# Channel attention and a Strassen-Winograd FFN: products chained in two PSUM banks, output blocks handled singly, token sums made by adding DMAs

## The reference

```python
qn = q / (np.linalg.norm(q, axis=1, keepdims=True) + 1e-06)
kn = k / (np.linalg.norm(k, axis=1, keepdims=True) + 1e-06)
s = kn.transpose(0, 2, 1) @ qn / tau
a = softmax(s)                       # over the last axis, 1e-9 added to the sum
x = (v @ a).reshape(12032, 256)
h = x @ w_in                         # w_in (256, 2048)
g = h * (1.0 / (1.0 + np.exp(-h)))
out = g @ w_out                      # w_out (2048, 256)
```

## Time and profile before

| | |
|---|---|
| median of 3 runs | 1074.42 us (1074.38 to 1074.58) |
| span of the profiled execution | 1072.1 us |
| PE busy | 1067.7 us, 4848 matmuls |
| VectorE busy | 730.0 us |
| ScalarE busy | 633.9 us |
| GpSimd busy | 62.0 us |
| DMA | 54.08 MB, mean 50 GB/s |

### The profile page before, as it was taken

One profiled execution on the slowest core, in us unless ns is written; L12 is line 12 of the kernel. 1 busy time (PEld: TensorE's weight loads), 2 busy tenths in 40 slices (PEclk: granted clock), 3 DMA queues, 4 the chain that ended last, 5 costly groups with the idle time before them and its releaser, 6 DMA issues.

```text
span 1072.1 us, 13055 instructions
## 1 busy us (share of the span) xinstructions
PE 1067.7 (100%) x4848; PEld 902.5 (84%) x4848; DVE 730.0 (68%) x941; ACT 633.9 (59%) x789; POOL 62.0 (6%) x33
## 2 busy tenths in 40 slices
PE   9999999999999999999999999999999999999998
PEld 8988888888888888888999888888888888888998
DVE  6889787567566566566788776667567566566665
ACT  7998665555555555555666655555555555555554
POOL 3792000000000000000000000000000000000000
PEclk9999999999999999999999999999999999999999
DMA  9991000200200200200200200200200200200100
GB/s 358 397 362 40 1 1 1 79 1 1 79 1 0 78 0 0 73 0 0 79 1 1 74 1 1 79 1 1 79 1 1 78 0 0 73 0 0 40 1 35
DMA packets 26365, 54.08 MB, mean 50 GB/s; under 512 B 2512, under 2 KB 6864, under 8 KB 26320
## 3 DMA queue, kind: packets, MB, share of 16 engines
q1 hardware_dynamic: 25888, 52.86, 13.5%
q10 hardware_dynamic: 432, 0.62, 0.2%
HBM read 41.16 MB, written 12.32 MB: 50 GB/s over the span
## 4 chain that ended last, share of the span: by engine, by line
PE 99%; DMA 0%; SPq 0%; ACT 0%; issue 0%
PE ps_o L530 16%; PE ps_o L531 16%; PE ps_o L529 16%; PE ps_h L496 14%; PE ps_h L495 14%; PE ps_h L494 14%; PE ps_o L434 5%; PE ps_o L449 1%; PE ps_o L456 1%; DMA qk<-k_dram 0%; PE ps_h L486 0%; PE ps_h L488 0%; PE ps_h L487 0%; PE ps_o L487 0%; PE ps_o L486 0%; PE ps_o L488 0%
## 5 line engine op out<-in xcount | busy, mean ns | idle before, releaser
L496 PE MATMUL ps_h<-b_hi,a_lo_rest 128*128 128x512 f32 (+1 forms) x504 | 194.1, 385 | 0.0
L495 PE MATMUL ps_h<-b_lo,a_hi_rest 128*128 128x512 f32 (+1 forms) x504 | 194.1, 385 | 0.0
L494 PE MATMUL ps_h<-b_hi,a_hi_rest 128*128 128x512 f32 (+1 forms) x504 | 194.0, 385 | 0.0
L978 DVE TENSOR_TENSOR h_b<-ps_h,u 128x512 f32<-128x512 f32 x96 | 66.4, 692 | 162.2 <-PE ps_h L496 162.1
L956 DVE TENSOR_TENSOR u<-ps_h,u 128x512 f32<-128x512 f32 x96 | 66.4, 692 | 142.4 <-PE ps_h L496 91.2
L750 ACT ACTIVATE h_a<-ps_h 128x512 f32<-128x512 f32 x96 | 57.4, 598 | 162.6 <-PE ps_h L496 162.6
L530 PE MATMUL ps_o<-g_lo_a,wo_hi 128*128 128x512 f32 (+1 forms) x384 | 147.9, 385 | 0.0
L529 PE MATMUL ps_o<-g_hi_b,wo_hi 128*128 128x512 f32 (+1 forms) x384 | 147.9, 385 | 0.0
L531 PE MATMUL ps_o<-g_hi_b,wo_lo 128*128 128x512 f32 (+1 forms) x384 | 147.9, 385 | 0.0
L529 PE MATMUL ps_o<-g_hi_a,wo_hi 128*128 128x512 f32 (+1 forms) x384 | 147.9, 385 | 0.0
L530 PE MATMUL ps_o<-g_lo_b,wo_hi 128*128 128x512 f32 (+1 forms) x384 | 147.8, 385 | 0.0
(11 more groups left out here) (138 smaller groups left out, 1602.1 us busy)
## 6 DMA issues: line engine op xcount, KB each, us to landing
v_raw<-v_t_dram SPq DMA_DIRECT2D x40, 256.0 KB, 3.7
out_t_dram<-v_raw SPq DMA_DIRECT2D x20, 512.0 KB, 3.2
qk<-q_dram SPq DMA_DIRECT2D x17, 384.0 KB, 10.8
qk<-k_dram SPq DMA_DIRECT2D x17, 384.0 KB, 11.8
wp_raw<-q_dram SPq DMA_DIRECT2D x7, 384.0 KB, 10.4
wp_raw<-k_dram SPq DMA_DIRECT2D x7, 384.0 KB, 11.8
w_in_raw<-w_in_dram SPq DMA_DIRECT2D x4, 512.0 KB, 11.8
wo_raw<-w_out_dram SPq DMA_DIRECT2D x4, 512.0 KB, 12.3
```

The lines of the kernel that those rows point to most:

```text
L494: nc.tensor.matmul(ps_h[:, bank, 0:n], w_hi, x_hi, start=start, stop=False, skip_group_check=True)
L495: nc.tensor.matmul(ps_h[:, bank, 0:n], w_hi, x_lo, start=False, stop=False, skip_group_check=True)
L496: return nc.tensor.matmul(ps_h[:, bank, 0:n], w_lo, x_hi, start=False, stop=stop, skip_group_check=True)
```

## The change

**Products.** p1 goes into bank X. ScalarE copies bank X into bank Y, still in PSUM ("seed"). p6 is then added upon p1 in bank X and gives U; p2 is added in bank Y and gives C11. ScalarE copies U out of bank X, p5 is added upon it and gives W, which is copied too, and p3 upon that gives the negative of C12. p7 starts bank Y anew; VectorE adds W and gets the negative of C22. p4 is added there, and VectorE adds U: C21. The signs of the weight sums are turned for it, and Silu takes a scale of -1 where the block is negative. Two of VectorE's five adds of a PSUM bank are left.

**Output blocks.** Each of C11, C12, C21 and C22 has its own tile, its own Silu, rounding, split and semaphores (`hi`, `lo`, `used`), and each output block of 3 matmuls stands alone between the products. The output banks are copied out one at a time at pairs 0 and 1.

**Token sums.** All token sums are now pure additions. For step 0 GpSimd makes them as before; for the others SP loads seven tiles of `x_raw` instead of four, and GpSimd issues seven DMAs that add a block of `v_t` from DRAM to a tile, in three rounds with a wait between.

**Code.** The loops over the steps are written out. In the last step of a batch ScalarE and VectorE take 448 columns in place of 512.

```diff
-BANK_P1, BANK_P6, BANK_P5, BANK_P7 = range(4)
+BANK_X, BANK_Y = range(2)
...
             def load_v(step):
+                places = ((T3, 0, 1), (B11, 0, 0), (B21, 1, 0), (B22, 1, 1))
+                if step:
+                    places += ((T1, 0, 0), (T2, 0, 0), (T4, 0, 0))
...
+            def add_tokens(step):
...
+                pool.wait_ge(v_loaded, 112 * step + 64)
+                add(T4, 0, 1).then_inc(t_first, 16)
+                add(T2, 0, 1).then_inc(t_first, 16)
+                add(T1, 0, 1).then_inc(t_first, 16)
+                add(T3, 1, 1).then_inc(t_first, 16)
+                pool.wait_ge(t_first, 64 * step)
+                add(T4, 1, 1).then_inc(t_second, 16)
+                add(T2, 1, 1).then_inc(t_second, 16)
+                pool.wait_ge(t_second, 32 * step)
+                add(T4, 1, 0).then_inc(t_third, 16)
...
+                p1(n, pair, par, tok)
+                output(n - 1, 0, 0, H12)
+                output(n - 1, 1, 0, H22)
+                p6(n, pair, par, tok)
+                p2(n, pair, par, tok)
+                output(n - 1, 0, 1, H12)
+                p5(n, pair, par, tok)
+                output(n - 1, 1, 1, H22)
+                p7(n, pair, par, tok)
+                output(n - 1, 0, 0, H11)
+                p3(n, pair, par, tok)
+                output(n - 1, 1, 0, H21)
+                p4(n, pair, par, tok)
+                output(n - 1, 0, 1, H11)
+                output(n - 1, 1, 1, H21)
+
+            def opening_pair():
+                pe.wait_ge(v_split, 3)
+                pe.wait_ge(a_split, 1)
+                p1(0, 0, 0, TOK)
+                pe.wait_ge(probs_split, 2)
+                fold(1, 0)
+                fold(1, 1)
+                p6(0, 0, 0, TOK)
+                p2(0, 0, 0, TOK)
+                fold(1, 2)
+                p5(0, 0, 0, TOK)
+                fold(1, 3)
...
+            def seed_u1(n, tok):
+
+                act.wait_ge(p1_done, n + 1)
+                if n:
+                    act.wait_ge(c21_made, n)
...
+                nc.scalar.activation(ps_h[:, BANK_Y, 0:tok], ps_h[:, BANK_X, 0:tok], ACT.Copy).then_inc(u1_seeded, 1)
...
+            def pair_step(n):
...
+                if n > 1:
+                    silu_c21(n - 1, before)
+                round_h(n - 1, before, H21, silu_21)
+                seed_u1(n, tok)
+                if it and pair == 0:
+                    copy_out(it - 1, 1, 0)
+                if it and pair == 1:
+                    copy_out(it - 1, 0, 1)
+                if it == 0 and pair < PAIRS - 1:
+                    round_a(0, pair + 1)
+                if it < ALL - 1 and pair == 3:
+                    round_t12(it + 1, 1 - par)
+                if it < ALL - 1 and pair == 4:
+                    round_v(it + 1, 1 - par)
+                if it < ALL - 1 and pair == 6:
+                    round_t34(it + 1, 1 - par)
+                copy_u(n, tok)
+                silu_c11(n, tok)
+                copy_w(n, tok)
+                if it and pair == 0:
+                    copy_out(it - 1, 1, 1)
+                silu_c22(n, tok)
+                silu_c12(n, tok)
+                round_h(n, tok, H22, silu_22)
+                round_h(n, tok, H12, silu_12)
+                if it and pair == 0:
+                    copy_out(it - 1, 0, 0)
+                round_h(n, tok, H11, silu_11)
+                place = n - PAIRS * (STEPS - 1)
+                if place in reload_at:
+                    old = reload_at[place]
+                    act.wait_ge(p4_done, PAIRS * (STEPS - 1) + old + 1)
+                    round_a(1, old)
...
+                make_c22(n, tok)
+                split_h(n, tok, H22)
+                if n == 0:
+                    split_wo(PARTS - 1)
+                make_c21(n, tok)
+                split_h(n, tok, H12)
+                if it == 0 and pair < PAIRS - 2:
+                    sum_a(0, pair + 2)
```

More of the change, by code:

```diff
@@ L36 @@
 FACTORS = 7
-BANK_P1, BANK_P6, BANK_P5, BANK_P7 = range(4)
+BANK_X, BANK_Y = range(2)
+H11, H12, H21, H22 = range(4)
 def channel_attention_ffn(nc, q, k, v_t, tau, w_in, w_out, out_t):
@@ L323, in _ @@
                 n = tokens_of(step)[1]
-                for late, t in enumerate((1, 0)):
-                    sp.wait_ge(out_copied, 2 * step + late + 3)
+                for t in (1, 0):
+                    for c in range(CK):
+                        sp.wait_ge(out_copied[CK * t + c], step + 1)
                     sp.dma_start(out_half(step, t), out_sb[:, t, :, 0:n]).then_inc(out_stored, 16)
@@ L424, in _ @@
             split_t34()
+            for step in range(1, ALL):
+                add_tokens(step)
         @block.tensor
@@ L580, in _ @@
-            for free in (o1_done, o2_done):
-                pe.sem_inc(free, 1)
+                x_hi, x_lo = b_hi[par][:, t, 0:tok], b_lo[par][:, t, 0:tok]
+                out = ps_h[:, bank, 0:tok]
+                nc.tensor.matmul(out, w_hi, x_hi, start=start, stop=False, skip_group_check=True)
+                nc.tensor.matmul(out, w_hi, x_lo, start=False, stop=False, skip_group_check=True)
+                return nc.tensor.matmul(out, w_lo, x_hi, start=False, stop=True, skip_group_check=True)
@@ new lines, in p4, with output @@
+            def p4(n, pair, par, tok):
+                pe.wait_ge(c22_made, n + 1)
+                product(pair, par, tok, BANK_Y, A22, T4, False).then_inc(p4_done, 1)
+            def output(n, f, c, g, stop=False):
+                it, pair = divmod(n, PAIRS)
+                tok = tokens_of(it)[1]
+                t = g % 2
+                if f == 0 and pair == 0:
+                    if it:
+                        pe.wait_ge(out_copied[CK * t + c], it)
+                    else:
+                        pe.wait_ge(wp_copied, 2 * FOLDS)
+                        pe.wait_ge(wo_split, PARTS)
+                pe.wait_ge(lo[g], n + 1)
+                block_, d = 2 * pair + f, slice(c * P, (c + 1) * P)
+                out = ps_o[:, CK * t + c, 0:tok]
+                last = pair == PAIRS - 1 and f == 1
+                nc.tensor.matmul(out, wo_hi[:, block_, d], g_hi[:, g, 0:tok], start=(pair == 0 and f == 0), stop=False,
+                                 skip_group_check=True)
+                nc.tensor.matmul(out, wo_hi[:, block_, d], g_lo[:, g, 0:tok], start=False, stop=False,
+                                 skip_group_check=True)
+                mm = nc.tensor.matmul(out, wo_lo[:, block_, d], g_hi[:, g, 0:tok], start=False, stop=last,
+                                      skip_group_check=True)
+                if c == 1:
+                    mm.then_inc(used[g], 1)
+                if c == 0 and last:
+                    mm.then_inc(out_summed[t], 1)
@@ L583, in _, with closing_outputs @@
+            def closing_outputs(n):
+                output(n, 0, 0, H12)
+                output(n, 1, 0, H22)
+                output(n, 0, 1, H12)
+                output(n, 1, 1, H22)
+                output(n, 0, 0, H11)
+                output(n, 0, 1, H11)
+                output(n, 1, 0, H21)
+                output(n, 1, 1, H21)
             pe.wait_ge(consts_made, 1)
@@ new lines, in silu_c12, with silu_c22, silu_c21 @@
+            def silu_c12(n, tok):
+                act.wait_ge(p3_done, n + 1)
+                if n:
+                    act.wait_ge(lo[H12], n)
+                nc.scalar.activation(h[:, H12, 0:tok], ps_h[:, BANK_X, 0:tok], ACT.Silu, scale=-1.0).then_inc(
+                    silu_12, 1)
+            def silu_c22(n, tok):
+                act.wait_ge(c22_made, n + 1)
+                nc.scalar.activation(h[:, H22, 0:tok], h[:, H22, 0:tok], ACT.Silu, scale=-1.0).then_inc(silu_22, 1)
+            def silu_c21(n, tok):
+                act.wait_ge(c21_made, n + 1)
+                nc.scalar.activation(h[:, H21, 0:tok], h[:, H21, 0:tok], ACT.Silu).then_inc(silu_21, 1)
```

533 lines of the change are left out of this document (221 added, 312 removed).

## The result

The changed kernel takes 1177.11 us (median of 4 runs, 1173.12 to 1183.39), the kernel before 1074.40 in the same series: a ratio of 1.096, interval 1.093 to 1.100. Forecast were 1085.3 and a range of 1079 to 1118. The direction was right, the size was too small by a factor of nine, and the range did not hold it.

The account below looks back on a forecast made before the run. The prediction held the feed-forward part bound by TensorE's matmul pace, so the change could only open gaps. Terms 6.9 + 1.1 + 1.7 + 1.2 + 0 = 10.9 us on 1074.4 gave 1085.3 us, range 1079 to 1118.

Parts of the forecast that it names:

- the sums made by DMAs: Token sums of eleven steps by adding DMAs: two rounds take 9.1 us at plain-load pace, 10.5 available, cost nought.
- the far bound, 77 us: Adds at twice the plain-load time, 18.2 us, cost 7.7 us in each of ten steps.
- the deadline of 33.0: Latest time into a step, in us, for ScalarE to begin rounding T1 and T2.
- the rival: Adds land late: 13.6 us, 3 late in each of ten steps, blocking ScalarE and p5; 30 us, 1115 us; chance 0.30.
- Reload: Second batch's weight roundings on ScalarE delay the seed copy and p6 at eight pairs, 0.85 us each: 6.9 us.
- The wide pair: Steady wide pairs: room 0.08 us before p6 and 0.01 before H12's first output; cost nothing.
- a rival at 0.12: Wide pairs stall too: 0.1 us missing in each of 79 pairs, 8 us more, 1093 us; chance 0.12.
- the narrow pairs: From p3's reader to the split of H12, 0.05 to 0.07 us late, 16 times: 1.1 us.
- Step 0's roundings: A weight rounding ahead of token roundings delays the copy of u for p5: 0.25, 0.25 and 0.67, sum 1.2 us.
- The opening: First pair: fold waits 1.0 us for the probabilities, late last folding copy 0.7; sum 1.7, between 1.0 and 3.
- Not slower: Rival: all waits met if ScalarE passes between instructions some 0.9 us a pair sooner; 1074 to 1076 us; chance 0.05.
- faster: Rival: fewer PSUM reads shorten the matmul pace by 3 ns each, 13 us, giving 1072 us; chance 0.03.

Follow-up runs that it names:

- hold10: Changed kernel without the adding DMAs, with ten extra 512-column ScalarE copies before the rounding of T1 and T2 in ten steps: 1175.19 us, ratio 1.094.
- Before_adds: Kernel before, loops written out, with the change's seven loads and seven adding DMAs a step in place of VectorE's token sums: 1088.55 us, ratio 1.014.
- mended: Changed kernel, T1/T2 rounded two pairs later, eight weight roundings behind the next seed copy, C22's first output block before C12's: 1087.65 us, ratio 1.012.
- seed_first: mended with ScalarE's seed copy moved ahead of the rounding of H21: 1085.18 us, ratio 1.010.

## Why the prediction failed, step by step

**The failed step: the sums made by DMAs, costed at nought.** The prediction bounded two rounds of adds between 9.1 and 18.2 us, allowed them 10.5, and took "the near end, nought, since the nearest row is the plain load of the same bytes". Measured are 15.8. Two things went wrong in this one step, the time of the rounds and the price of being late, and a third was right.

First the choice of the end. The nearest row moved the same bytes with another operation, and only the lowest 1.4 us of a range of 9.1 fitted the budget of 10.5. Even plain copies from GpSimd take 6.31 + 3.92 = 10.2, which the row's 9.1 had already missed by 1.1. With no row for an operation, and a penalty on one side only, nought was the edge of the range, not its middle. The prediction had worked out the far bound, 77 us, and given late adds 0.30, but left that part out of its range. The budget was slightly too large as well: the loads had landed 23.7 us into step 1 (213.00 less the step's start near 189.3, which is the p1 of its fourth pair at 219.90 less the 30.6 of three) where 22.5 was forecast, while ScalarE stood ready at 228.58 - 6.79 = 221.79, or 32.5, half a microsecond before the deadline of 33.0. From 23.7 to 33.0 are 9.3 us, and 15.8 is 6.5 late; the gap in PE there is 6.1, ScalarE's wait 6.8. So the arithmetic of the rival was right: with 15.8 in place of its 13.6 it gives 53 us by the budget of 10.5 and 65 by that of 9.3, and the ten gaps sum to 60.3. Its own middle, 1115 us, was still 62 below the measured time.

The Trainium skill's rule from "Collectives: The Full Stack", "The bandwidth ceiling: the fold count and why AG ≠ RS ≠ AR", that an add reads twice for each write and runs near half rate (there it is the reducing step of a ring of cores), was set against the row and lost. The runs side with it: the packets take twice the time for the same bytes (2030 against 989 us), and the rounds, latency and issue included, 1.5 and 1.6 times that of plain copies. That the second read is the reason is not shown: the adds also go in smaller packets, though plain packets of that size took 0.092 us and not 0.206.

Second, the rival counted each late microsecond as one of PE, but no more. PE lost a further 21 us in ten steps to the half clock behind the gaps, which hold10 shows to be an effect of the gap alone. The prediction's rows had a granted clock of 1.00, in a stretch where PE never stood; a price per gap could not be read there. The Trainium skill does have the effect: "TensorE: Matmul & The Clock Gate", "HAM oscillation — how this bites in real kernels", says that a PE that waits for a transfer in each tile resumes at the lower clock every time. The trace agrees: a granted clock of 0.50 behind each gap of 4 us or more, and 0.427 us from one wide matmul to the next.

Third, and right: lateness would not be absorbed. PE stood for 59.2 of ScalarE's 66.7 us. Before_adds shows that this belongs to the chained order; in the order before the same 65.9 cost 9.8.

**Reload, 6.9 us: right.** Eight gaps of 0.80 to 0.87 before p6, 6.7 us, between 561 and 712 us (515 to 660 were forecast, without the late adds); moving the roundings gave back 6.1. The timeline at the fifth of them shows p6 waiting for the seed copy of 512 columns, 0.58 us long where 0.60 was taken:

```profile
640.60 0.58 ACT L743 ACTIVATE ps_h<-ps_h 128x512 f32<-128x512 f32 x1
...
641.23 0.49 PE L508 MATMUL ps_h<-b_hi,a_hi_first 128*128 128x512 f32 x1 [0.71 <-ACT ps_h L743]
```

**The wide pair, costed at nothing: mis-sized.** Rooms of 0.01 and 0.08 us were rounded to "free", with the loss of 8 us as a rival at 0.12. The remainder of 9 us, with the narrow pairs for which 1.1 was forecast, sits nearer to that rival. Two of its causes are shown by taking them away in turn: mended and seed_first together gave 4.7 us. In mended, one wait's removal uncovered the next, as two rooms near nought should lead one to expect.

**Step 0's roundings, 1.2: right, measured 1.3.** Three gaps before p5 as forecast, of 0.19, 0.62 and 0.19 for 0.25, 0.67 and 0.25, and 0.11 more behind each.

**The opening, 1.7: measured 4.3.** The fold's wait was right in kind (1.0 forecast, 1.3 measured), and so was the late copy near the end (0.7 against 1.0). Of the missing 2.6 us, 1.7 lie ahead of the FFN, where I had looked at no row: its first matmul starts at 97.57 after, against 95.89 before. 1.0 of them has a reason told in the last section; the other 0.7 is within what differs there from run to run.

**The other rivals.** "Not slower" and "faster" fell: no steady pair had room, and the matmul pace did not shorten with fewer reads of PSUM (0.2280 on average, and in seed_first, with as few reads, the spacings of before).

## What to carry to other kernels

When PE is full, a change can only open gaps, so cost every new wait by its slack, and count a gap of some microseconds at more than its length: here 7.9 us for one of 5.9, since the matmuls behind it ran at half clock. Where an operation has no row, do not take the end of its range that happens to fit the budget; keep the far end in what you forecast, or put the work where either end fits, as moving one rounding by two pairs did here for 81 us. A chain in few banks turns every late releaser into a stall, and two queues with near-zero slack must be mended together, because the second takes over when the first is gone.
